# Attention and mixing with query tiles of 128, 128, 128, 96 and 96 rows instead of 128, 128, 128, 128 and 64

## The reference

```python
B, H, S, D = 4, 8, 576, 64          # batches, heads, sequence, head width
q_rot, k_rot = rotate(q), rotate(k) # rotary position encoding
scores = q_rot @ k_rot.T / sqrt(D)  # 576 x 576 for each of the 32 heads
attn = exp(scores - max(scores))
attn = attn / (sum(attn) + 1e-9)
x = (attn @ v) with the 8 heads of a batch side by side      # B x 576 x 512
u = x + ((x.T @ U) @ V).T           # U: 576 x 32, V: 32 x 576, mixing along the sequence
out = u + relu(u @ w_ch1) @ w_ch2   # 512 -> 2048 -> 512, rows independent
```

## Time and profile before

| | |
|---|---|
| median of 3 runs | 755.5 us (755.38 to 759.19) |
| profiled execution | 755.52 us |
| its span, first to last instruction | 753.7 us |
| TensorE busy | 712.1 us (94%), 4292 matmuls, granted clock 1.00 |
| PEld busy | 640.9 us (85%), overlaps PE |
| GpSimd busy | 465.4 us (62%) |
| ScalarE busy | 438.8 us (58%) |
| VectorE busy | 407.8 us (54%) |
| DMA | 117.82 MB, 156 GB/s |

### The profile page before, as it was taken

One profiled execution on the slowest core, in us unless ns is written; L12 is line 12 of the kernel. 1 busy time (PEld: TensorE's weight loads), 2 busy tenths in 40 slices (PEclk: granted clock), 3 DMA queues, 4 the chain that ended last, 5 costly groups with the idle time before them and its releaser, 6 DMA issues.

```text
span 753.7 us, 12305 instructions
## 1 busy us (share of the span) xinstructions
PE 712.1 (94%) x4292; PEld 640.9 (85%) x4292; DVE 407.8 (54%) x676; ACT 438.8 (58%) x948; POOL 465.4 (62%) x338
## 2 busy tenths in 40 slices
PE   3999987899999989999999999899999999999998
PEld 2888875799998879999999988788999889898986
DVE  5799997655556775344444566666555441112111
ACT  2788876676666666565565665667656343434341
POOL 4898865585668664664946867628433346565653
PEclk9999999999999999999999999999999999999999
DMA  7777675537474438348274373462623254434342
GB/s 208 196 210 201 190 208 153 179 95 207 129 228 134 140 126 246 131 144 241 85 220 165 103 209 131 139 191 79 160 70 107 69 196 137 165 128 168 127 167 72
DMA packets 73756, 117.82 MB, mean 156 GB/s; under 512 B 27040, under 2 KB 27168, under 8 KB 71904
## 3 DMA queue, kind: packets, MB, share of 16 engines
q1 hardware_dynamic: 73472, 116.68, 51.2%
q10 hardware_dynamic: 224, 0.36, 0.2%
HBM read 80.15 MB, written 9.44 MB: 119 GB/s over the span
## 4 chain that ended last, share of the span: by engine, by line
PE 75%; DVE 10%; ACT 7%; issue 5%; POOL 1%; DMA 1%; POOLq 0%; SPq 0%; ACTq 0%; DVEq 0%
PE ps L1131 25%; PE ps L1147 23%; PE ps L1045 8%; PE ps L1031 8%; PE ps L1065 6%; DVE negmax L865 3%; ACT prob L711 2%; PE ps L1058 1%; DVE ptl L874 1%; PE ps L1023 1%; ACT pth L722 1%; PE ps L1088 1%; DVE pth L878 1%; DMA raw<-in_qk 1%; PE ps L1113 1%
## 5 line engine op out<-in xcount | busy, mean ns | idle before, releaser
L650 POOL TENSOR_TENSOR w2l<-w2u,w2h 128x512 fp32r<-128x512 f32 x96 | 123.9, 1291 | 227.6 <-ACT w2h L775 227.6
L966 DVE SCALAR_TENSOR_TENSOR htl<-ps,hth 128x384 fp32r<-128x384 f32 x96 | 53.6, 558 | 183.9 <-ACT hth L782 183.6
L865 DVE TENSOR_REDUCE negmax<-ps 128x1 f32<-128x576 f32 (+1 forms) x160 | 120.2, 751 | 54.7 <-PE ps L1031 45.1
L711 ACT ACTIVATE prob<-ps,negmax 128x576 f32<-128x576 f32 (+1 forms) x160 | 117.9, 737 | 35.7 <-DVE negmax L865 34.4
L722 ACT ACTIVATE pth<-ps 128x512 fp32r<-128x512 f32 x156 | 87.5, 565 | 82.7 <-PE ps L1065 80.8
L1131 PE MATMUL ps<-ub,w1h 128*128 128x384 f32 x384 | 132.4, 345 | 2.2 <-DVE utl L957 2.2
L1131 PE MATMUL ps<-ub,w1l 128*128 128x384 f32 x384 | 129.5, 337 | 0.0
L1131 PE MATMUL ps<-utl,w1h 128*128 128x384 f32 x384 | 129.3, 337 | 0.0
L644 POOL TENSOR_TENSOR w1l<-w1u,w1h 128x512 fp32r<-128x512 f32 x96 | 123.7, 1289 | 6.7 <-ACT w1h L771 6.7
L782 ACT ACTIVATE hth<-ps 128x384 fp32r<-128x384 f32 x96 | 47.0, 490 | 136.9 <-PE ps L1131 136.7
L1031 PE MATMUL ps<-stack 128*128 128x288 f32 x620 | 113.3, 305 | 10.0 <-ACT prob L711 9.6
(11 more groups left out here) (81 smaller groups left out, 1127.0 us busy)
## 6 DMA issues: line engine op xcount, KB each, us to landing
w1u<-in_w SPq DMA_DIRECT2D x96, 256.0 KB, 2.6
w2u<-in_w SPq DMA_DIRECT2D x96, 256.0 KB, 2.6
stack<-raw SPq DMA_DIRECT2D x60, 288.0 KB, 4.5
raw<-in_qk SPq DMA_DIRECT2D x14, 1152.0 KB, 5.8
stack<-raw SPq DMA_DIRECT2D x60, 144.0 KB, 4.0
v2u<-in_v SPq DMA_DIRECT2D x16, 320.0 KB, 3.9
ubu<-scratch_u SPq DMA_DIRECT2D x18, 256.0 KB, 3.5
out<-ubu SPq DMA_DIRECT2D x18, 256.0 KB, 2.2
```

Source lines behind the costliest of these rows:

```text
L650: nc.gpsimd.tensor_tensor(w2l[:, at], w2u[:, at], w2h[:, at], ALU.subtract).then_inc(w2_lo, 1)
L711: nc.scalar.activation(tile_of(n, WT[t]).rearrange("p (c n) -> p c n", c=2), scores_of(n, WT[t]), ACT.Exp, bias=negmax[0:WT[t], t:t + 1], ...
L865: nc.vector.tensor_reduce(negmax[0:WT[t], t:t + 1], scores_of(n, WT[t]), AX.XY, ALU.max, negate=True).then_inc(maxed, 1)
```

## The change

The query tiles become 128, 128, 128, 96 and 96 rows; their starts are now in a table `QO` = 0, 128, 256, 384, 480 instead of 128 t. The key tiles stay as they are (`KW` = 64 is the width of the last). Unit 3 turns a tile of 96 queries, LAST one of 96 as well (5 x 96 = 480 columns of a bank), TAIL covers 480 queries, three transposes of 128 and one of 96. In batch 3, "pair" takes the query tiles 0 to 2 and "pair_end" 3 and 4. U is laid out by the new tiles. `slot_ns` and `part_ns` and with them the dealing out of the MLP parts are untouched.

```diff
-WT = [min(P, S - P * t) for t in range(NT)]
+KW = S - P * (NT - 1)
+FULL = 3
+WT = [P] * FULL + [(S - P * FULL) // (NT - FULL)] * (NT - FULL)
+QO = [sum(WT[:t]) for t in range(NT)]
+TURNED = QO[NT - 1]
...
         if j == TAIL:
-            return bank.rearrange("p (c n) -> p c n", c=1)[0:D], slice(NT - 1, NT), slice(0, BANK)
+            return bank[:, 0:TURNED].rearrange("p (c n) -> p c n", c=1)[0:KW], slice(NT - 1, NT), slice(0, TURNED)
         if j == LAST:
             return (bank[:, 0:NT * WT[-1]].rearrange("p (c n) -> p c n", c=NT), slice(0, NT),
-                    slice(P * (NT - 1), S))
-        return bank.rearrange("p (c n) -> p c n", c=NT - 1), slice(0, NT - 1), slice(P * j, P * j + P)
+                    slice(TURNED, S))
+        return (bank[:, 0:(NT - 1) * WT[j]].rearrange("p (c n) -> p c n", c=NT - 1), slice(0, NT - 1),
+                slice(QO[j], QO[j] + WT[j]))
...
-        rows, tiles = (P, slice(0, NT - 1)) if what == "pair" else (WT[-1], slice(NT - 1, NT))
+        rows, tiles = (P, slice(0, FULL)) if what == "pair" else (WT[-1], slice(FULL, NT))
...
                                               stack[:, g % HEADS_STACKED, 0, QO[t]:QO[t] + WT[t]],
...
                     for t in range(NT - 1):
-                        mm = nc.tensor.transpose(bank[:, 0, P * t:P * t + P],
-                                                 prob[:, S * t + P * (NT - 1):S * t + S], ident[:, :])
+                        mm = nc.tensor.transpose(bank[:, 0, QO[t]:QO[t] + WT[t]],
+                                                 prob[0:WT[t], S * t + P * (NT - 1):S * t + S],
+                                                 ident[0:WT[t], 0:WT[t]])
...
-                        _, tiles, hi, lo = x_parts("pair" if i < NT - 1 else "pair_end", t)
+                        _, tiles, hi, lo = x_parts("pair" if i < FULL else "pair_end", t)
```

More of the change, by code:

```diff
@@ L101 @@
 UT = 2 * S
-UT_NEEDED = [NT * ((TB * (p + 1) - 1) // S) + ((TB * (p + 1) - 1) % S) // P + 1 for p in range(NB)]
+UT_NEEDED = [NT * ((TB * (p + 1) - 1) // S) + sum(at <= (TB * (p + 1) - 1) % S for at in QO) for p in range(NB)]
 PARTS = [("up", 0, 0), ("up", 0, 1)]
@@ L308, in build @@
         v2u, v2 = sb_over("v2", "v2u", [P, 2, NT, 2, 2, D])
-        prob = sb("prob", [P, NT * S + P - WT[-1]])
+        prob = sb("prob", [P, NT * S + P - KW])
         pth = sb("pth", [P, NT, S], F32R)
@@ L423, in ut_cols @@
     def ut_cols(b, t):
-        at = S * (b % 2) + P * t
+        at = S * (b % 2) + QO[t]
         return slice(at, at + WT[t])
@@ L488, in store_u @@
                 sp.wait_ge(u_ready, b * NT + t + 1)
-                at = S * b + P * t
+                at = S * b + QO[t]
                 sp.dma_start(scratch_u[at:at + WT[t], :], xn[0:WT[t], t]).then_inc(u_stored, 16)
@@ L762, in mix @@
                     if b >= 2:
-                        act.wait_ge(up_done, FB * ((S * (b - 2) + P * t + WT[t] - 1) // TB + 1))
+                        act.wait_ge(up_done, FB * ((S * (b - 2) + QO[t] + WT[t] - 1) // TB + 1))
                     nc.scalar.activation(uth[:, :, ut_cols(b, t)],
@@ L1023, in scores @@
                             mm = nc.tensor.matmul(ps[0:WT[t], at + c * BANK:at + c * BANK + CH],
-                                                  first[0:D, 0, q, 0, P * t:P * t + WT[t]],
+                                                  first[0:D, 0, q, 0, QO[t]:QO[t] + WT[t]],
                                                   first[0:D, 0, k, 1, CH * c:CH * c + CH],
@@ L1031, in scores @@
                         mm = nc.tensor.matmul(ps[0:WT[t], at + c * BANK:at + c * BANK + CH],
-                                              stack[:, g % HEADS_STACKED, 0, P * t:P * t + WT[t]],
+                                              stack[:, g % HEADS_STACKED, 0, QO[t]:QO[t] + WT[t]],
                                               stack[:, g % HEADS_STACKED, part, CH * c:CH * c + CH],
@@ L1078, in mix @@
                         mm = nc.tensor.transpose(work(tenant, 0, rows, DM)[:, columns(i - tiles.start)],
-                                                 xt_of(b, t)[:, P * i:P * i + rows], ident[:, :])
+                                                 xt_of(b, t)[:, QO[i]:QO[i] + rows], ident[:, :])
                     mm.then_inc(nat_done, 1)
@@ L1094, in mix @@
                         mm = nc.tensor.transpose(work(tenant, 0, rows, DM)[:, P * c:P * c + P],
-                                                 xt_of(b, c)[:, P * t:P * t + rows], ident[:, :])
+                                                 xt_of(b, c)[:, QO[t]:QO[t] + rows], ident[:, :])
                     mm.then_inc(nat_done, 1)
@@ L1106, in mix @@
                     pe.wait_ge(h_ready, all_of(HIDDENS, b))
-                    mm = nc.tensor.matmul(work(tenant, 0, rows, DM), vs[:, P * t:P * t + rows], hs[:, :],
+                    mm = nc.tensor.matmul(work(tenant, 0, rows, DM), vs[:, QO[t]:QO[t] + rows], hs[:, :],
                                           start=True, stop=True)
@@ L1200 @@
     vp = np.ascontiguousarray(vp.reshape(B * PAIRS, NT, P, 2, D).transpose(0, 2, 1, 3, 4))
-    u4 = np.zeros((SP_, 4, R), moe_U.dtype)
-    u4[:S] = moe_U[:, None, :]
-    u4 = np.ascontiguousarray(u4.reshape(NT, P, P).transpose(1, 0, 2))
+    u4 = np.zeros((P, NT, 4, R), moe_U.dtype)
+    for t in range(NT):
+        u4[:WT[t], t] = moe_U[QO[t]:QO[t] + WT[t], None, :]
+    u4 = u4.reshape(P, NT, P)
     v4 = np.ascontiguousarray(np.concatenate([moe_V] * 4, axis=0))
```

## The result

| | before | changed |
|---|---|---|
| first comparison, median (range) | 755.56 us (755.37 to 759.19, 6 runs) | 751.17 us (748.61 to 752.65, 6 runs) |
| second comparison, median (range) | 756.06 us (755.16 to 758.78, 9 runs) | 749.43 us (748.49 to 751.16, 5 runs) |
| ratio, first (95% interval) | | 0.9925 (0.9898 to 0.9951) |
| ratio, second (95% interval) | | 0.9907 (0.9887 to 0.9926) |
| runs with granted clock 1.00, second comparison | 755.76 us (5 of 9) | 748.70 us (3 of 5) |

The change makes the kernel faster, by 4 to 7 us where 10.5 were forecast. The medians of both kernels hold runs in which TensorE was granted 1.2 GHz instead of 2.4 in some stretches; the number of these differs from run to run of the same kernel, so the size of the effect is read from runs at clock 1.00: 7.1 us in the second comparison (755.76 - 748.70).

The account below looks back on a forecast made before the run. TensorE was taken to bound the kernel behind 150 us, VectorE's sum the first regime. Gains 0.2 + 6.8 + 1.4 + 1.4 + 0.7 + 0.6 = 11.1 us, less 0.6: 755.52 - 10.5 = 745.0 us, range 742.5 to 750.

Parts of the forecast that it names:

- 64-row border: At LAST and pair_low, 64 active rows lose about 0.34 to 0.35 us per block; 96 rows were taken to lose nothing.
- What is freed around the blocks: TensorE gains: LAST 6.8 us, transpose columns 0.2, turned_u of tile 4 1.4, pair_low 1.4, "low" of tile 4 0.7.
- Columns trade one for one: Unit 3, LAST and TAIL trade columns: transposes gain 0.2 us, ScalarE and VectorE nothing in sum.
- A faster TensorE comes earlier to waits whose chains are not its own; I take 0.6 off: At TensorE's waits for exponentials, x splits and weights: 0.6 us of the summed gain is lost.
- The sign that the sum of waits should stay below 12 us: TensorE's waits between 150 and 700 us, 9 us before, should stay below 12; rival B would add 7 for exponentials.
- pair and pair_end pass a tile's columns from one to the other in a serial chain, again nothing: At pair and pair_end, a tile's 128 columns only move from one to the other; no time gained or lost.
- The shorter turned_u of tile 3: It shrinks from 512 to 384 columns, shortening the longest L957 wait and one at 139.7 us; 0.6 us together.
- First regime: Before 97 us VectorE's sum decides; head periods stay about 8.7 us, bounds -1.5 to +1.2 us.
- A: Any change in active rows costs a border, so 96 rows pay as 64 do: +15.8, 771 us; chance 8%.
- B: Slots are paced by scores, maximum, exponential; freed 0.34 us becomes waiting for the exponential: 752 to 755 us; chance 7%.
- C: 96 rows lose about half of what 64 lose, neighbouring units too; gain and loss about cancel, 750 to 757 us; 5%.

Follow-up runs that it names:

- the second profile: Second profiled execution of the unaltered changed kernel, clock 1.000 throughout; span 747.6 us against 753.7 of the kernel before.
- the moved version: Changed kernel with pair_low of pairs 1 and 2 one slot later (146 and 156 instead of 145 and 155); 750.13 us, ratio 0.9909.
- the first profile: Profiled execution of the unaltered changed kernel in the first comparison; 750.79 us, span 749.0, clock 0.995.

## Why the prediction was right in its mechanism and too large

- **The reading of the 64-row border held.** LAST block 1.11 us (1.09 forecast), unit 3 and TAIL 1.48 (1.46), no border at the entry to 96 rows, pair_low's ten matmuls evenly 0.11 apart. The experiment with one 64-row matmul gives the same 0.33.
- **What is freed around the blocks was taken a little too large.** From slot 60 on it is 8.7 us, where 6.8 + 0.2 + 1.4 + 0.7 and three of the four turned_u (1.0) make 10.1 in the sum. A head gives 0.30 us (0.20 + 0.10) and not 0.34 and a bit more: two hundredths are missing at each of its two 96-row units. The prediction took the whole 0.34 beyond the columns as the border, but a few hundredths of it stay with a last transpose of fewer columns. The turned_u of tile 4 gives 0.24 for 0.34, "low" 0.19 for 0.34, pair_low 0.29 for 0.35.
- **Columns trade one for one: held.** Transposes are 0.082 apart at 96 columns, by the columns alone.
- **The step that failed is "A faster TensorE comes earlier to waits whose chains are not its own; I take 0.6 off".** The waits behind slot 60 took 3.4 us in the second profile, about 0.7 less in an execution with the shorter L1086 wait. The term was sized beside a total of waits of 9 us in the trace before. That total says how late TensorE's partners are now; it does not say how many are nearly late. In about ten places, most of them at mixing items, TensorE newly waits or waits 0.2 us or more longer: the store of u ahead of the first pair (+1.1, of which 0.6 comes back because a wait for the exponential behind it is gone), the residual (+0.5), two pair_low (0.5 and 0.4, gone when they are moved), and others with 0.2 to 0.4 each. The sign that the sum of waits should stay below 12 us held (11.3 from 9.1), and yet more than five times what was taken off was lost: the sum of waits grew by 2.2 us, the start-to-start distances by 3.4.
- **"pair and pair_end pass a tile's columns from one to the other in a serial chain, again nothing" is right only for the last pair.** In the pairs 0 to 2, pair_end stands alone in its slot ahead of pair_low, and it is pair_end that grows (128 to 256 columns in three instructions). That this widening itself was waited for is argued from the order; the moved version does not separate it from the bank.
- **The shorter turned_u of tile 3**: its waits shrank by 0.15 and 0.11 us where 0.3 each was forecast (1.41 to 1.26 at 140 us, 1.40 to 1.29 at 488).
- **First regime**: VectorE's sum decides, as forecast; its head takes 8.61 us instead of 8.69, within the bounds.
- **Not foreseen: the granted clock.** It falls in both kernels. Of the miss of 6.2 us (751.17 - 745.0) it makes 2.6, the distance of the first median from that comparison's one run at clock 1.00 (748.61). The other 3.6 us are the waits (2.7 to 3.4 where 0.6 was taken off and 0.3 each expected back at two places) and the blocks (1.4 too much), against a little more from the stretch up to slot 60. No part of the 3.6 is measured in that one run, which has no trace; the split is that of the second profile.
- Rivals: A is refuted by the 0.53 us at entry; B too, since the exponential's waits did not grow; but its form, freed time that turns into waiting, was right at the mixing items. C is refuted: a 96-row unit loses a few hundredths (0.03 at LAST) and not half of 0.34.

## What to carry to other kernels

Read TensorE from start to start and compare the intervals where the active rows change: in this kernel 64-row operands between full-height ones cost a third of a microsecond for each visit, and a tile of 96 rows does not. When a busy engine gets faster, list the waits that are nearly late (the chains that end within a few tenths before their user) and not only those that already show, above all where a small ring of banks ties a rare item to a unit that the change makes wider. An instruction that lasts longer in one place than in another (hs) may be a wait for another engine that the profile counts as busy. And compare runs by granted clock before believing a difference of half a percent.

## What the runs showed of the hardware

- A visit to 64 active rows costs 0.33 to 0.34 us beyond its columns in the experiment and at the LAST units. A change in active columns (128*64, 128*96) costs nothing that the trace shows, and a change to 96 rows a few hundredths of a microsecond at most. TensorEngine Tiling (Array Packing) in the Trainium skill, Key Properties, names a drain at each change of mode: the loss at 64 rows fits that, though no run shows that it is a drain, and at 64 columns no loss is seen.
- The clock of TensorE fell to half in stretches of 3.4 us (118 to 121 us and 135 to 138 in the first profile) behind waits near 112 to 121, 135 and 593 to 602 us, in about half of the runs of either kernel, while TensorE was fully busy in the stretch itself (3.00 of 3.00 us). Where it falls on the MLP it costs 1.5 us.
- VectorE's hs instruction of 32x512 elements took 0.78 to 3.02 us, ending each time 0.55 us behind the GpSimd instruction that was running when it started. It stands on the chain of the residual.
